# Slots' outputs times the last stage's first matrix in four 32-column tiles, experts interleaved, output weights split piece by piece

## What is computed

```python
logits = x @ phi                                   # 3072 x 32
slot_input = softmax(logits, over tokens).T @ x    # 32 slots x 384
for e in range(8):                                 # 4 slots each
    h = np.maximum(slot_input[e] @ w1[e], 0.0)     # 384 -> 1024
    slot_out[e] = h @ w2[e]                        # 1024 -> 384
x = softmax(logits, over slots) @ slot_out         # 3072 x 384
h = np.maximum(x @ w_in, 0.0)                      # 384 -> 2048
out = h * h @ w_out                                # 2048 -> 384
```

## Time and profile before

| | us |
|---|---|
| median of 3 runs | 705.66 |
| lowest, highest | 704.86, 709.02 |
| profiled execution | 709.5 |
| its span in the trace | 707.8 |
| busy: TensorE, its weight loads | 529.5, 401.9 |
| busy: VectorE, ScalarE, GpSimd | 403.1, 327.2, 157.9 |

### The profile page before, as it was taken

How to read it: one execution, slowest core, us unless ns; L and a number is a source line. 1 busy time by engine, 2 the same in 40 slices (tenths; PEclk the granted TensorE clock), 3 DMA queues, 4 the chain that set the end, 5 groups by cost and what they waited for, 6 DMA issues and landing times.

```text
span 707.8 us, 11711 instructions
## 1 busy us (share of the span) xinstructions
PE 529.5 (75%) x4544; PEld 401.9 (57%) x4544; DVE 403.1 (57%) x661; ACT 327.2 (46%) x555; POOL 157.9 (22%) x131
## 2 busy tenths in 40 slices
PE   1000009796597975969787987897999999999997
PEld 1000006575375754657576863445888888888885
DVE  1399995899699996969643315034333323333331
ACT  4867043363655826313132341244565655565553
POOL 5001000100001000010000000057555555555553
PEclk9999999898699988979898999999999999999999
DMA  6030082553636333668799696920010100000011
GB/s 237 2 132 0 2 213 65 114 123 80 196 96 131 106 80 79 129 196 252 134 237 263 137 426 260 425 103 1 2 45 1 44 2 34 11 15 31 1 45 44
DMA packets 39558, 79.59 MB, mean 112 GB/s; under 512 B 7120, under 2 KB 28752, under 8 KB 37200
## 3 DMA queue, kind: packets, MB, share of 16 engines
q1 hardware_dynamic: 36192, 62.33, 31.0%
q10 hardware_dynamic: 3312, 16.52, 7.1%
HBM read 55.12 MB, written 4.72 MB: 85 GB/s over the span
## 4 chain that ended last, share of the span: by engine, by line
PE 48%; DVE 21%; DMA 10%; ACT 7%; SPq 5%; issue 5%; POOL 3%; ACTq 0%; DVEq 0%; POOLq 0%
PE ps L1200 9%; PE ps L1202 9%; PE ps L1201 9%; PE ps L954 7%; DMA stk<-xout 7%; SPq L248 4%; DMA wouts<-in_w_out 3%; PE ps L1184 3%; PE ps L940 2%; DVE tt L666 2%; DVE xout L762 2%; DVE big L671 2%; DVE tt L668 2%; SPq L258 2%; PE ps L994 2%
## 5 line engine op out<-in xcount | busy, mean ns | idle before, releaser
L924 DVE TENSOR_TENSOR qs<-rs 128x512 f32<-128x512 f32 x96 | 70.0, 730 | 147.7 <-ACT rs L548 147.7
L613 POOL TENSOR_TENSOR hlo<-qs,hhi 128x512 fp32r<-128x512 f32 x96 | 124.7, 1300 | 92.4 <-DVE qs L924 89.4
L940 PE MATMUL ps<-ident 128*32 128x512 bf16 x260 | 76.0, 399 | 90.6 <-DMA stk<-xout 90.6
L954 PE MATMUL ps<-stk 112*128 112x224 f32 (+1 forms) x384 | 92.7, 408 | 54.2 <-DMA stk<-xout 38.3
L954 PEld LDWEIGHTS ps<-stk 112*128 112x128 f32 x384 | 82.0, 236 | 66.3 <-DMA stk<-xout 43.2
L1200 PE MATMUL ps<-hhi,who 128*128 128x512 f32 x288 | 112.8, 392 | 4.0 <-POOL hlo L613 4.0
L1202 PE MATMUL ps<-hhi,wlo 128*128 128x512 f32 x288 | 112.5, 391 | 0.0
L1201 PE MATMUL ps<-hlo,who 128*128 128x512 f32 x288 | 112.5, 391 | 0.0
L548 ACT ACTIVATE rs<-ps 128x512 f32<-128x512 f32 x96 | 57.4, 598 | 95.6 <-PE ps L1184 95.4
L940 PEld LDWEIGHTS ps<-ident 128*32 128x32 bf16 x260 | 21.0, 98 | 113.0 <-DMA stk<-xout 90.9
L598 POOL MEMSET big<- 128x2304 f32 x4 | 8.1, 2037 | 286.1 <-DVE big L671 286.1
(11 more groups left out here) (146 smaller groups left out, 825.8 us busy)
## 6 DMA issues: line engine op xcount, KB each, us to landing
stk<-xout SPq DMA_DIRECT2D x144, 128.0 KB, 3.7
wt<-in_w SPq DMA_DIRECT2D x10, 1536.0 KB, 11.9
xq<-in_xq SPq DMA_DIRECT2D x24, 384.0 KB, 4.8
wt<-in_w ACTq DMA_DIRECT2D x6, 1536.0 KB, 8.6
big<-in_a_all ACTq DMA_DIRECT2D x9, 768.0 KB, 7.1
vr<-in_v_all SPq DMA_DIRECT2D x24, 192.0 KB, 4.1
out<-ost SPq DMA_DIRECT2D x6, 768.0 KB, 3.5
wins<-in_w_in SPq DMA_DIRECT2D x1, 3072.0 KB, 17.7
```

The source lines that it names most:

```text
L613: pool.tensor_tensor(hlo[:, i % NHS, :], qs[:, i % NQS, :], hhi[:, i % NHS, :].bitcast(F32), ALU.subtract).then_inc(lo_ready, 1)
L924: dve.tensor_tensor(qs[:, i % NQS, :], rs[:, i % NQS, :], rs[:, i % NQS, :], ALU.mult).then_inc(sq_ready, 1)
L940: nc.tensor.matmul(ps[P - SL:P, 7, :], idb[:, 0:SL], idle, start=True, stop=True)
L954: last = nc.tensor.matmul(ps[:, h // 2, h % 2 * SK:h % 2 * SK + cols], x[:, 0:CH], x[:, CH:CH + cols], start=True, stop=True)
```

## The change

The experts' blocks are reordered on TensorE (a hidden block two pairs ahead of its slot outputs, transposes of c between them) and VectorE's first `hts` copy moves ahead of the four casts of c. The places of the sixteen expert matrices are permuted (`W_AT`) so that both w1 places of pair 0 are free after `hidden(0)`, and those of `w_in` and `w_out` after `hidden(1)` and `hidden(2)`; SP's waits follow. `so` is stored once, its product with `w_in` runs as four 32-column matmuls, one for each 512 columns of `w_in`, all into one bank; ScalarE copies the result to `ub`, and four matmuls with 32 rows of a 0/1 matrix (`sel4`) spread each group to 128 partitions in a bank of its own. ScalarE stores all 128 partitions rounded, and VectorE subtracts in place in the lower half, without `uhi`. The split of the output weights becomes sixteen pieces of 384 columns, one ahead of each of the first sixteen steps on ScalarE and VectorE; GpSimd has no part in it. `gate` and `project` wait for their pieces only. Eight idle matmuls ahead of the third gate become four.

```diff
         NW = 14
-        wt = [place(f"wt{k}", [P, KM * FE], offset=k % NW * WT) for k in range(2 * NX)]
+        W_AT = [0, 4, 1, 5, 2, 6, 3, 7, 8, 10, 9, 11, 12, 13, 0, 1]
+        EARLY = [W_AT.index(k) for k in range(6)]
+        wt = [place(f"wt{k}", [P, KM * FE], offset=W_AT[k] * WT) for k in range(2 * NX)]
         at[0] = NW * WT
         sinz = place("sinz", [P, KM, NX, SL])
...
-        so4 = place("so4", [P, KM, 4, SL])
+        so = place("so", [P, KM, SL])
+        sel4 = place("sel4", [P, 4, SL])
+        ub = place("ub", [P, TW])
         assert at[0] <= after_at, (at[0], after_at)
         wins = place("wins", [P, KM, F2], offset=2 * WT)
-        wlo = place("wlo", [P, F2B, DM], F32R, offset=4 * WT)
-        wouts = place("wouts", [P, F2B, DM], offset=4 * WT)
-        who = place("who", [P, F2B, DM], F32R, offset=6 * WT)
-        cst = place("cst", [P, B * S], F32R, offset=8 * WT)
-        at[0] = 9 * WT
+        wlo = place("wlo", [P, F2B, DM], F32R, offset=8 * WT)
+        wouts = place("wouts", [P, F2B, DM], offset=8 * WT)
+        who = place("who", [P, F2B, DM], F32R, offset=4 * WT)
+        cst = place("cst", [P, B * S], F32R, offset=6 * WT)
+        at[0] = 10 * WT
         NQS, NHS = 3, 4
         ust = place("ust", [P, F2], F32R)
-        uhi = place("uhi", [P, 2, TW], F32R)
         qs = place("qs", [P, NQS, TW])
         hhi = place("hhi", [P, NHS, TW], F32R)
         hlo = place("hlo", [P, NHS, TW], F32R)
         ost = place("ost", [P, 2, KM, TW])
         rs = place("rs", [P, NQS, TW])
-        assert at[0] <= NW * WT
+        assert at[0] <= NW * WT + 4 * (KM * NX * SL + NT * 4 * SL)
+        U_BANK = [5, 6, 1, 7]
...
-            for k in range(6, 9):
+            for k in (8, 5, 7):
                 load_w(k)
             sp.wait_ge(stacked[(NT - 1) % NST], 96 * ((NT - 1) // NST + 1))
             for k in (10, 9):
                 load_w(k)
             sp.wait_ge(y_done, NT)
-            for k in range(11, NW):
+            for k in (12, 11, 13):
                 load_w(k)
-            sp.wait_ge(o_done, 1)
-            for k in range(NW, 2 * NX):
+
+            sp.wait_ge(h_done, 1)
+            for k in (14, 15):
                 load_w(k)
+            sp.wait_ge(h_done, 2)
             sp.dma_start(wins[:], w_in).then_inc(ld_win, 16)
-            sp.wait_ge(o_done, 2)
+            sp.wait_ge(h_done, 3)
             sp.dma_start(wouts[:], w_out).then_inc(ld_wout, 16)
...
-                        load_w(c - 2)
+                        load_w(EARLY[c - 2])
                     if p == B and c < 3:
                         if c == 0:
                             act.wait_ge(chain, C_ALL * B)
                             act.wait_ge(kq_ready, 2 * NC * (B - 1))
-                        load_w(3 + c)
+                        load_w(EARLY[3 + c])
...
-                    act.wait_ge(o_done, 3)
+                    act.wait_ge(o_done, 2)
...
-            def split_w(k):
-                if k == 0:
+            def split_w(f):
+                if f == 0:
                     act.wait_ge(ld_wout, 16)
-                    act.wait_ge(o_done, 2)
-                q = slice(F2B // 4 * k, F2B // 4 * (k + 1))
-                nc.scalar.activation(who[:, q], wouts[:, q], ACT.Copy).then_inc(wo_high, 1)
+                    act.wait_ge(o_done, 1)
+                nc.scalar.activation(who[:, f], wouts[:, f], ACT.Copy).then_inc(wo_high, 1)
 
             relu_h(0)
             relu_h(1)
             relu_h(2)
+            relu_h(3)
+            for b in range(TT):
+                copy_c(b)
+            act.wait_ge(u_done, 1)
+            nc.scalar.activation(ub[:], ps[:, 0, :], ACT.Copy).then_inc(ub_ready, 1)
             for b in range(4):
-                copy_c(b)
-            relu_h(3)
-            copy_c(4)
-            copy_c(5)
-            for b in range(4):
-                split_w(b)
-            for b in range(4):
-                act.wait_ge(u_done, b + 1)
-                if b == 0:
-                    act.wait_ge(o_done, NP)
-                nc.scalar.activation(ust[0:R1, b * TW:(b + 1) * TW], ps[0:R1, b, :], ACT.Copy).then_inc(u_high, 1)
+                act.wait_ge(u_done, b + 2)
+                nc.scalar.activation(ust[:, b * TW:(b + 1) * TW], ps[:, U_BANK[b], :], ACT.Copy).then_inc(u_high, 1)
             for i in range(TT * F2B + 1):
+                if i < F2B:
+                    split_w(i)
...
-                pool.wait_ge(wo_high, k + 1)
-                q = slice(F2B // 4 * k, F2B // 4 * (k + 1))
-                pool.tensor_tensor(wlo[:, q], wouts[:, q], who[:, q].bitcast(F32), ALU.subtract).then_inc(wo_low, 1)
+            pool.wait_ge(sin_ready, 1)
+            pool.tensor_copy(sel4[:], bass.AP(sel, 0, [list(sel[:].ap[0]), [0, 4], [1, SL]])).then_inc(sin_zero, 1)
...
+            def copy_h(p):
+                dve.wait_ge(ht_done, p + 1)
+                if p >= 2:
+                    dve.wait_ge(o_done, p - 1)
+                dve.tensor_copy(hts[p % 2][:], ps[:, 1 if p % 2 else 4, :]).then_inc(h_ready, 1)
+
+            copy_h(0)
             step(dve.tensor_copy(c4[:, :, 0, :], cexp[:]), False)
             step(dve.tensor_copy(c4[:, :, 2, :], cexp[:]))
             step(dve.tensor_tensor(c4[:, :, 1, :], cexp[:], c4[:, :, 0, :].bitcast(F32), ALU.subtract), False)
             step(dve.tensor_tensor(c4[:, :, 3, :], cexp[:], c4[:, :, 0, :].bitcast(F32), ALU.subtract))
             assert done[0] == C_READY, done[0]
 
-            for p in range(NP):
-                dve.wait_ge(ht_done, p + 1)
-                if p >= 2:
-                    dve.wait_ge(o_done, p - 1)
-                dve.tensor_copy(hts[p % 2][:], ps[:, 1 if p % 2 else 4, :]).then_inc(h_ready, 1)
+            for p in range(1, NP):
+                copy_h(p)
 
             dve.wait_ge(o_done, NP)
             dve.tensor_copy(rows_o[:], ps[:, 5, 0:DM]).then_inc(rows_ready, 1)
             dve.wait_ge(o_done, NP + 1)
-            o = ps[:, 4, 0:KM * SL]
-            ob = bass.AP(ps, o.offset, [list(o.ap[0]), [SL, KM], [0, 4], [1, SL]])
-            dve.tensor_copy(so4[:], ob).then_inc(so_ready, 1)
+            dve.tensor_copy(so[:], ps[:, 4, 0:KM * SL].rearrange("p (k s) -> p k s", k=KM)).then_inc(so_ready, 1)
             for b in range(4):
-                dve.wait_ge(u_done, b + 1)
-                if b >= 2:
-                    dve.wait_ge(u_low, 2 * b - 2)
-                dve.tensor_copy(uhi[R1:P, b % 2, :], ps[R1:P, b, :]).then_inc(u_low, 1)
-                dve.wait_ge(u_low, 2 * b + 1)
-                dve.tensor_tensor(ust[R1:P, b * TW:(b + 1) * TW], ps[R1:P, b, :], uhi[R1:P, b % 2, :].bitcast(F32),
-                                  ALU.subtract).then_inc(u_low, 1)
+                dve.wait_ge(u_high, b + 1)
+                low = ust[R1:P, b * TW:(b + 1) * TW]
+                dve.tensor_tensor(low, ps[R1:P, U_BANK[b], :], low.bitcast(F32), ALU.subtract).then_inc(u_low, 1)
...
+                    dve.wait_ge(wo_high, i + 1)
+                    dve.tensor_tensor(wlo[:, i], wouts[:, i], who[:, i].bitcast(F32), ALU.subtract).then_inc(wo_low, 1)
...
             transpose_h(0)
+            hidden(2)
             slot_outputs(0)
             transpose_h(1)
+            hidden(3)
             slot_outputs(1)
-            hidden(2)
             transpose_h(2)
+            pe.wait_ge(soft, C_READY)
+            transpose_c(0)
+            transpose_c(1)
             slot_outputs(2)
-            pe.wait_ge(soft, C_READY)
-            for b in range(4):
-                transpose_c(b)
-            hidden(3)
+            transpose_h(3)
+            transpose_c(2)
+            transpose_c(3)
+            slot_outputs(3)
             transpose_c(4)
-            transpose_c(5)
-            transpose_h(3)
-            slot_outputs(3)
             pe.wait_ge(rows_ready, 1)
             gather_rows().then_inc(o_done, 1)
-            keep_busy(3)
+            transpose_c(5)
             pe.wait_ge(so_ready, 1)
             pe.wait_ge(ld_win, 16)
+            for k in range(KM):
+                for b in range(4):
+                    last = nc.tensor.matmul(ps[SL * b:SL * (b + 1), 0, :], so[:, k, :], wins[:, k, b * TW:(b + 1) * TW], start=(k == 0),
+                                            stop=(k == KM - 1))
+            last.then_inc(u_done, 1)
+            keep_busy(3)
+            pe.wait_ge(sin_zero, 2)
+            pe.wait_ge(ub_ready, 1)
             for b in range(4):
-                if b == 2:
-                    pe.wait_ge(ct_copied, 6)
-                for k in range(KM):
-                    last = nc.tensor.matmul(ps[:, b, :], so4[:, k].rearrange("p q s -> p (q s)"),
-                                            wins[:, k, b * TW:(b + 1) * TW], start=(k == 0), stop=(k == KM - 1))
-                last.then_inc(u_done, 1)
+                nc.tensor.matmul(ps[:, U_BANK[b], :], sel4[SL * b:SL * (b + 1)].rearrange("p q s -> p (q s)"),
```

(25 more changed lines are left out.)

6 lines of the change are left out of this document (2 added, 4 removed).

## The result

| | before | changed |
|---|---|---|
| median, us | 707.34 (4 runs) | 688.34 (4 runs) |
| lowest, highest | 704.86, 709.24 | 686.96, 691.24 |
| ratio, 95% interval | | 0.9748 [0.9713, 0.9784] |
| profiled execution, its span | 709.5, 707.8 | 689.7, 687.8 |
| attention, up to the `sinz` instruction | 428.6 | 426.7 |

The kernel became 2.5% faster; 688.8 us were forecast. That forecast stood on a median before of 705.66 us (3 runs), which a fourth run moved to 707.34. The spans differ by 20.0 us, but 1.9 of them are the attention, which wasn't touched. `sinz`, VectorE's last instruction ahead of the first hidden matmul, divides the two: from there to the end it is 18.1 us less.

A forecast was written before the change was run, and what follows sets the result against it. Last stage bound by TensorE's matmuls, its start by waits for the output-weight load and split. project(0) earlier -16.0, clock -1.4, blocking +0.5: -16.9 us off the 705.66 median gives 688.8 us; range 685 to 694.

The forecast's parts named there:

- Loads: Last expert matrices and weights: issued earlier, the queue never runs dry; output weights land at 459.8 instead of 466.6 us.
- TensorE's order: Reordered expert blocks from 434.46 us: slot_outputs(3) starts at about 452.3, input-weight matmuls at 457.3 us.
- The 0.2 us held for matrix 14: Expert blocks: hidden(3) might wait some 0.2 us because matrix 14 comes at 441.0 us; counted in TensorE's order.
- the 4.99 us: From slot_outputs(3) to the input-weight matmuls (`rows_o`, gather, `so`): 4.99 us in the earlier trace, kept for the new order.
- The other end of this cost: Spreading matmuls on 32-row tiles: if one after the other, 3.4 us instead of 0.9, and project(0) at 468.8, 0.7 later.
- The clock: Head of the last stage: longest TensorE hole 2.0 us, so the clock holds at 2.4 GHz, -1.4 us.
- VectorE and GpSimd: First sixteen steps: two-input SBUF work excludes GpSimd's; a step takes 2.25 us, under TensorE's 2.27; cost +0.5 us.
- The rival with more than 0.5: First sixteen steps: GpSimd and VectorE block each other for +1 to +4 us, giving 690 to 693; chance 0.2.
- the other order of the prediction: First sixteen steps: if `wlo` always arrives during `hlo`, a step takes 2.53 us, 0.26 too long.
- The cushion of 1.6 us: Last stage: `hlo` ends at 493.10 and is wanted at 494.69, 1.6 us later, which absorbs part of any blocking.
- the bounds of 2.6 and 4.3 us: First sixteen steps: largest blocking loss after the cushion, 2.6 us; with full durations and handing over (2.64 a step), 4.3.
- the other signs: Wrong if `wlo` or `hlo` well over 0.6 and 1.3 us with TensorE idle, clock 0.5 after 467, or hidden(3) waiting.

The follow-up runs named there:

- two-input op added: Changed kernel plus one VectorE subtraction of 384 columns, both inputs in SBUF, in each of the first sixteen steps: stage 267.0 us, ratio 0.9818.
- PSUM copy ahead: Changed kernel plus a VectorE copy of 384 columns from PSUM ahead of the `wlo` subtraction in the first sixteen steps: stage 265.5 us, ratio 0.9784.
- late loads: Changed kernel with the last two expert matrices and the input weights issued after slot_outputs(0) again: stage 271.9 us, ratio 0.9845.
- pieces on GpSimd: Changed kernel with the sixteen `wlo` subtractions on GpSimd, ahead of each `hlo`, instead of VectorE: stage 269.7 us, ratio 0.9837.
- the changed kernel once more: The changed kernel itself, unedited, run again beside three others on the same chip: stage 263.5 us, ratio 0.9703.

## Why the prediction was right

- **Loads.** Forecast: no gap, matrix 14 at 441.0, the output weights at 459.8. With the 1.9 us by which the attention ended earlier, that is 439.1 and 457.9; measured 438.9 and 457.2.
- **TensorE's order.** Input-weight matmuls forecast at 28.7 us behind `sinz` (457.3), measured 28.1. The 0.2 us held for matrix 14 weren't needed in this execution; in three others it was 0.2, 0.2 and 0.9. Another 0.3 is the narrower copy to `so` (0.26 instead of 0.56 us), which I had left in the 4.99 us. No run puts the old order of the experts back, so this part rests on the traces: in the kernel before, TensorE's holes between hidden(1) and these matmuls add up to 7.1 us (the largest 2.83), in the changed kernel none is listed.
- **Input-weight matmuls.** Forecast 2.84 us to the reader, measured 457.65 - 454.80 = 2.85. The 32-row tiles do run abreast: eight records in 1.14 us against 3.4 one by one. The other end of this cost can be dropped.
- **project(0).** Forecast 39.5 us behind `sinz`, measured 38.9; that makes -16.6 instead of -16.0. The chain ran as told: four VectorE subtractions (2.52), `wlo` 0.56, `qs`, `hlo`.
- **The clock.** The term, -1.4, was right, but in part by luck: its reason was not shown, and runs speak against it. I compared the longest hole (2.0 us forecast, 1.6 measured) with one of 2.8 us that had kept the clock. Without the fillers the clock fell after holes of 0.8 and 1.4 us only, and with fillers and a hole of 2.0 us it fell once and held once. A single hole's length is not what decides; the fillers, which I costed at nothing, made 2.9 us in the one execution without them.
- **VectorE and GpSimd.** Forecast a round of 2.25 us and +0.5 us in all; measured 2.17, and no loss (222.2 against 223.7 - 1.4 = 222.3). The rival with more than 0.5 didn't happen, but it was close: a round has 0.10 us to spare, and one PSUM copy in the wrong place uses it up. That run shows the other order of the prediction, `wlo` arriving during `hlo` (2.53 forecast, 2.44 measured). The cushion of 1.6 us, which bounded the rival, was read off a step some 10 us behind project(0) and isn't there at the head, so the bounds of 2.6 and 4.3 us were 1.6 too low. Two readings of the earlier trace rows were slightly off, without effect on the sum beyond 0.03 us a step: that `qs` didn't end with `wlo` but 0.55 us behind it (482.86 and 482.31), which is the same handing over as behind `hlo`, and `hlo` ended 1.11 us behind `qs`, not 1.14.
- **Sum.** -16.9 forecast, -18.1 in the stage: 0.6 at project(0), 0.5 for the blocking, and a tenth of rounding. That the median came within 0.5 us of the forecast is partly chance: the medians differ by 19.0 us, and single executions of the changed kernel range from 686.96 to 691.24.
- **A sign that was set wrong.** The prediction names "a distance from project(0) to the end above 220 us" as a sign of being wrong. It is 222.2 us, and by the prediction's own sum it had to be above 220: 707.8 - 484.12 = 223.7, less 1.4, plus 0.5 is 222.8. The sign says nothing about the mechanism. Of the other signs, `hlo` did take 1.47 us and not 1.3, but TensorE wasn't idle; no load was late, and the clock stayed at 1.00.

## What to carry to other kernels

Follow every chain that ends at the same instruction to its own end: one part of this change was worth 4.6 us added alone and 15.5 us taken out of the finished kernel (some 11 to 15.5 by where it is put back), and no such number is "its" gain. When work moves from GpSimd to VectorE, count rounds and not busy time, and keep VectorE's instructions with two SBUF inputs side by side, with the others behind them. Where a fixed stage follows a noisy one, compare from a common instruction: here the noise ahead (7 us) was more than twice what leaving out the fillers cost.

## What the runs showed of the hardware

- A VectorE instruction with two SBUF inputs and GpSimd's subtraction exclude each other (`qs` 1.77 us instead of 0.69, `hlo` 1.48 instead of 1.29), and the one that starts first in the gap has the turn: a copy from PSUM between two such VectorE instructions hands it to GpSimd (rounds of 2.44 and 2.17 us, same work). The Trainium skill ("SBUF — State Buffer", two separate sides) has the exclusion and that whichever starts first gets the ports for its whole length, and the rows agree; what the order of VectorE's own instructions costs is from these runs.
- Four 32-row matmuls into four banks run side by side: eight f32 records of 512 columns in 1.14 us.
- The granted clock fell to 1.2 GHz when TensorE had just been busy for 1.8 of 4 us with no hole longer than 1.4 us, and had held through a hole of 2.8 us between busy stretches. Ahead of project(0), after the same instructions on TensorE and holes of 2.06 and 1.99 us, it held in one execution (two-input op added: 1.00) and fell in another (PSUM copy ahead: 0.63 in the next 3 us). What exactly decides stays open.
- In three of the executions (late loads, pieces on GpSimd, the changed kernel once more) TensorE came to the first hidden block at half clock (0.57 to 0.63 already in the 3 us ahead of `sinz`) and lost 2.4 to 2.6 us there, with the same instructions as in the others. Its busy time further ahead is the same in all fourteen executions (6.85 of the 8 us and 4.00 of the 4 us up to 6 us ahead of `sinz`), so that doesn't tell them apart; the cause stays open.
- A load of 1.5 MB landed 6.6 us (late loads) and 7.6 us (kernel before) after its issue into a queue that had moved nothing for over 2 us, and 3.6 to 3.8 us behind the one before it in a full one.
